# First two w_in blocks of the last layer: gates taken ahead of y's last tile and of waiting weight parts, w_out parts made first, output banks dealt out anew

## The chip, the cores and the metric

The kernel runs on one core of one Trainium2 chip. The metric is the device time of one execution in microseconds (us). Engines are named as in the profile: PE (TensorE, with its weight loads as PEld), DVE (VectorE), ACT (ScalarE), POOL (GpSimd) and SP (SyncE, which issues the transfers).

## The reference

Three stages follow each other. The change lies in the last one.

```
attn = masked softmax attention (2 x 8 heads, 768 positions, 64 wide)     -> x, 1536 x 512
h    = max(x @ w1, x @ w2, x @ w3)                                       1536 x 768
y    = h @ w_out                                                         1536 x 512
h2   = y @ w_in                                                          1536 x 2048
g    = h2 * sigmoid(1.702 * h2)
out  = g @ w_out2                                                        1536 x 512
```

## The kernel before

**Numbers as two parts.** Every matrix that PE multiplies is held as a high part (a rounded copy) and a low part (the number less its high part). One product is three matmuls: high by high, high by low, low by high. For each operand ACT (or POOL) makes the copy, and DVE (or POOL) the difference.

**y.** y is made in 16 tiles, n = 0 to 15 (two batches of 768 rows, four chunks, two halves), each into one of PSUM's banks 0 to 3 in turn. `y_hi(n)` on ACT (L863) copies the tile rounded, `y_raw_copy(n)` on ACT (L868) copies it plain, `y_lo(n)` on DVE (L1151) takes the difference, and after it the bank is free. The sixteenth, n = 15, is y's last tile.

**The last layer.** It goes through 16 blocks n (`MIXES`), eight slices of w_in for each batch. One block is a 2 x 2 block product done by a scheme with seven products in place of eight: `up2(n, 0)` to `up2(n, 6)` on PE (L1393 to L1395, six matmuls each), into two half banks in turn (banks 5 and 6), so that `up2` of product m waits until the product two before it has been read. What reads them:

- `first_copy(n)` on ACT (L900) copies product 0, and `mix(n, 0)` to `mix(n, 6)` on DVE (L1209) add products 1 to 6 up. Four of the mixes give the four tiles of h2.
- `sigmoid(n, w)` on ACT (L907), `gate(n, w)` on DVE (L1214), `g_hi(n, w)` on ACT (L914) and `g_lo(n, w)` on DVE (L1219), w = 0 to 3, make the tiles of g from them. sigmoid(n, 0) needs mix(n, 2), sigmoid(n, 1) mix(n, 4), sigmoid(n, 2) mix(n, 5), sigmoid(n, 3) mix(n, 6).
- `out2(n, u)` on PE (L1492 to L1494, three matmuls each), u = 0 to 11, multiplies g by w_out2 and adds into the six output tiles, which have a bank each in `acc`. The first three need g_lo(n, 0), the next three g_lo(n, 1), and so on. PE puts out2 of block n - 1 between the products of block n: `OUT_SPREAD` says how many behind each product (2, 2, 2, 2, 1, 2, 1). The tiles come in the order 3, 4, 5, 0, 1, 2, 3, 4, 5, 0, 1, 2.

The first block's products are made between y's last four tiles: up2(0, 5) and (0, 6) come right behind y's tile 15. Then come block 1 and its neighbours.

**The weights of a block.** w_in's slice is loaded by SP (L485) and POOL adds up four sums of its quarters (L669, named s1, s3, s2 and s4; s2 needs s1, s4 needs s2). The seven parts have a high and a low part: `in2_hi(n, w)` on ACT (L884; for blocks 0 and 1 POOL does it, L524) and `in2_lo(n, w)` on POOL (L678). Part 1 is s2, part 5 is s4. The two w_out2 slices of a block are loaded by SP (L491) and split by `out2_hi(g)` on ACT (L892) and `out2_lo(g)` on POOL (L683), g = 2n and 2n + 1.

**Orders.** All five engines run lists written out by hand, each in order, with semaphores between them. From block 2 on (and in the kernel before from block 1 on) ACT's list for block n is: sigmoid(n - 1, 3), first_copy(n), g_hi(n - 1, 3), in2_hi(n + 1, 1 to 4), out2_hi(2n) and (2n + 1), in2_hi(n + 1, 5 and 6), for n = 2 to 5 a copy `y_sum_hi` (L873), in2_hi(n + 2, 0), and then sigmoid and g_hi (n, 0 to 2). POOL's is: in2_lo(n + 1, 1 to 4), s4 of block n + 1, out2_lo(2n) and (2n + 1), in2_lo(n + 1, 5 and 6), and then s1, in2_lo(n + 2, 0), s3 and s2 of block n + 2. DVE's is: gate(n - 1, 3), g_lo(n - 1, 3), mix(n, 0), for n = 1 to 4 a sum `y_sum` (L1189), mix(n, 1), for n = 3 to 6 `y_sum_lo` (L1194), mix(n, 2), mix(n, 3), gate(n, 0), mix(n, 4), g_lo(n, 0), gate(n, 1), mix(n, 5), g_lo(n, 1), gate(n, 2), mix(n, 6), g_lo(n, 2).

For block 0 DVE's list behind y's tile 14 is: mix(0, 2 to 4), gate(0, 0), y_lo(15), g_lo(0, 0), gate(0, 1), mix(0, 5), g_lo(0, 1), mix(0, 6), gate(0, 2), g_lo(0, 2).

Of the kernel before, what the change touches and what calls it, by code (L numbers as in the profile page):

```python
# [5 lines left out]
def lsh_attention_ffn(nc, q, k, v, proj, w1, w2, w3, w_out, w_in2, w_out2, out):  # L6
# [5 lines left out]
    B, H, S, D = q.shape  # L12
# [87 lines left out]
    with ctx:  # L100
# [118 lines left out]
        all_banks = [psS[0][:, 0, :], psS[0][:, 1, :], psS[1][:, 0, :], psS[1][:, 1, :],  # L219
                     psR[0][:, :], psR[1][:, :], psR[2][:, :], psO[:, :]]  # L220
        psY = all_banks[0:4]
        acc = all_banks[0:4] + [psR[0][:, :], psO[:, :]]
        psU = [psR[1][:, 0:HALF], psR[2][:, 0:HALF]]

        consts_set = sem("consts_set")
# [287 lines left out]
        def _(pool):  # L513
# [167 lines left out]
            def out2_lo(g):  # L681
                pool.wait_ge(out2_hi_made, g + 1)
                pool.tensor_tensor(w2_parts[:, g % W2_SLOTS, 1, :], out2_raw(g), f32(w2_parts[:, g % W2_SLOTS, 0, :]),  # L683
                                   ALU.subtract).then_inc(out2_split, 1)
# [24 lines left out]
                in2_lo(n, 6)  # L709
            in2_first_sums(2)  # L710
            for n in range(1, MIXES):
                if n + 1 < MIXES:
                    for which in range(1, 5):
                        in2_lo(n + 1, which)
                    in2_last_sum(n + 1)
                out2_lo(2 * n)
                out2_lo(2 * n + 1)
                if n + 1 < MIXES:
                    in2_lo(n + 1, 5)
                    in2_lo(n + 1, 6)  # L720
                if n + 2 < MIXES:
                    in2_first_sums(n + 2)
# [3 lines left out]
        def _(act):  # L726
# [197 lines left out]
            for n in range(2 * OUTS * B):  # L924
                if n == 0:
                    act.wait_ge(h_lo_made, 2 * UPS)
                if n == 2 * OUTS:
                    act.wait_ge(h_lo_made, 2 * UPS * B)
                if n == 2 * OUTS * B - 6:
                    act.activation(table_probe[:, :], ident[:, 0:1], ACT.Sigmoid)  # L930
                if n == 2 * OUTS * B - 1:
                    sigmoid(0, 0)
                y_hi(n)
                y_raw_copy(n)
                if n in (2 * OUTS, 2 * OUTS + 1):
                    for t in T_ORDER2[2 * (n - 2 * OUTS):2 * (n - 2 * OUTS) + 2]:
                        y_sum_hi(0, t)
                if n == 2 * OUTS * B - 4:
                    first_copy(0)
                    out2_hi(0)  # L940
                    out2_hi(1)
            g_hi(0, 0)
            sigmoid(0, 1)
            g_hi(0, 1)
            sigmoid(0, 2)
            g_hi(0, 2)

            for n in range(1, MIXES):
                sigmoid(n - 1, 3)
                first_copy(n)  # L950
                g_hi(n - 1, 3)
                if n == FPS2 + 1:
                    copy_result(0, COPIES[0][2])
                if n == 1:
                    in2_hi(2, 0)
                if n + 1 < MIXES:
                    for which in range(1, 5):
                        in2_hi(n + 1, which)
                out2_hi(2 * n)
                out2_hi(2 * n + 1)  # L960
                if n + 1 < MIXES:
                    in2_hi(n + 1, 5)
                    in2_hi(n + 1, 6)
                if 2 <= n < 6:
                    y_sum_hi(1, T_ORDER2[n - 2])
                if n + 2 < MIXES:
                    in2_hi(n + 2, 0)
                for which in range(3):
                    sigmoid(n, which)
                    g_hi(n, which)  # L970
                if n == FPS2:
                    copy_result(0, COPIES[0][0])
                    copy_result(0, COPIES[0][1])
# [7 lines left out]
        def _(dve):  # L981
# [255 lines left out]
            mix(0, 3)  # L1237
            mix(0, 4)
            gate(0, 0)
            y_lo(2 * OUTS * B - 1)  # L1240
            g_lo(0, 0)
            gate(0, 1)
            mix(0, 5)
            g_lo(0, 1)
            mix(0, 6)
            gate(0, 2)
            g_lo(0, 2)
# [34 lines left out]
        def _(pe):  # L1282
# [195 lines left out]
            def out2(n, u):  # L1478

                b, (i, tile_) = n // FPS2, OUT_UNITS[u]  # L1480
                first, last = n % FPS2 == 0 and u < NT, n % FPS2 == FPS2 - 1 and u >= NT
                if u % TH == 0:
                    pe.wait_ge(g_lo_made, 4 * n + u // TH + 1)
                if u == 0:
                    pe.wait_ge(out2_split, 2 * n + 2)
                if first and b == 0:
                    pe.wait_ge(y_lo_made, 2 * OUTS * B)
                    pe.wait_ge(y_raw_made, 2 * OUTS * B)
                if first and b > 0:
                    pe.wait_ge(*result_done(b - 1, tile_))  # L1490
                wh, wl = w2_parts[:, (2 * n + i) % W2_SLOTS, 0, :], w2_parts[:, (2 * n + i) % W2_SLOTS, 1, :]
                pe.matmul(acc[tile_], g_part(n, i, 0)[:, ts(tile_, P)], wh, start=first, stop=False)  # L1492
                pe.matmul(acc[tile_], g_part(n, i, 0)[:, ts(tile_, P)], wl, start=False, stop=False)  # L1493
                pe.matmul(acc[tile_], g_part(n, i, 1)[:, ts(tile_, P)], wh, start=False, stop=last).then_inc(tile_summed, 1)  # L1494
# [52 lines left out]
```

## Time and profile before

| | us |
|---|---|
| median of 3 runs | 685.02 |
| lowest, highest | 684.53, 685.94 |
| the profiled execution, its own time | 683.02 |
| its span | 681.2 |
| PE busy | 665.6 |
| DVE busy | 493.1 |
| POOL busy | 475.6 |
| ACT busy | 342.7 |

The profile is of one execution. The span runs from its first to its last instruction; some 1.8 us of its own time lie around the span. Matmuls are pipelined: one of 384 columns is shown 0.33 us long, and the next starts about 0.17 us behind it. An engine's idle time stands in brackets behind the instruction that ended it, with the event that released it by the profile. Where several events were waited for, the one named may not be the last.

### The profile page before, as it was taken

The page shows a single profiled execution, that of the slowest core. Times are in us where ns is not written, and L with a number is a line of the kernel's source. Part 1 is how long each engine was busy: PE and PEld are TensorE (multiplying, and loading weights), DVE is VectorE, ACT ScalarE, POOL GpSimd, SP SyncE. Part 2 cuts the span into 40 slices and gives each one's busy share as a digit, 9 for nine tenths or more (in the row PEclk, how much of TensorE's full clock was granted, in tenths as well). Part 3 has the DMA queues.
Part 4 walks back from the last instruction along what each step waited for, and adds up shares of the span by engine and source line. Part 5 has one row for each costly group of instructions (what it writes and reads, how often), then busy time and mean ns, then how long its engine had stood idle before and what let it go on. Part 6 is the DMA issues. An engine that isn't in the chain of part 4 may idle for free.

```text
span 681.2 us, 11928 instructions
## 1 busy us (share of the span) xinstructions
PE 665.6 (98%) x3874; PEld 576.3 (85%) x3874; DVE 493.1 (72%) x971; ACT 342.7 (50%) x752; POOL 475.6 (70%) x542
## 2 busy tenths in 40 slices
PE   7899999999999999999999999989999999999998
PEld 5677777767777789999999999869989889898986
DVE  5778788787877799879788963566777666555554
ACT  3777877777777731011103453455555555545433
POOL 4756757688976899968870538888888767777720
PEclk9999999999999999999999999999999999999999
DMA  5845737548243101111010201122222115222102
GB/s 115 192 94 138 170 89 174 127 121 185 57 124 120 33 23 40 32 32 32 25 46 25 94 0 44 50 62 64 76 78 93 64 50 167 63 63 62 39 25 92
DMA packets 58701, 54.12 MB, mean 79 GB/s; under 512 B 28945, under 2 KB 47633, under 8 KB 58641
## 3 DMA queue, kind: packets, MB, share of 16 engines
q1 hardware_dynamic: 58320, 53.36, 29.1%
q8 instruction: 32, 0.52, 0.3%
q14 instruction: 29, 0.23, 0.1%
q10 hardware_dynamic: 320, 0.01, 0.0%
HBM read 32.51 MB, written 3.15 MB: 52 GB/s over the span
## 4 chain that ended last, share of the span: by engine, by line
PE 92%; DVE 2%; POOL 2%; DMA 1%; issue 1%; ACT 1%; SPq 0%; DVEq 0%; ACTq 0%; POOLq 0%
PE psS L1325 10%; PE psO L1347 9%; PE psR L1333 9%; PE psR L1393 8%; PE psR L1394 8%; PE psR L1395 8%; PE psS L1393 6%; PE psS L1394 6%; PE psS L1395 6%; PE psS L1494 4%; PE psS L1493 4%; PE psS L1492 4%; PE psR L1294 2%; PE psR L1494 1%; PE psR L1493 1%; PE psO L1493 1%
## 5 line engine op out<-in xcount | busy, mean ns | idle before, releaser
L549 POOL TENSOR_SCALAR probs<-probs,lone,inv 128x768 f32<-128x768 f32 x96 | 94.0, 986 | 60.2 <-DVE inv L1010 60.2
L678 POOL TENSOR_TENSOR w_lo<-w_raw,w_hi 128x256 fp32r<-128x256 f32 x96 | 79.7, 842 | 49.7 <-ACT w_hi L884 48.7
L992 DVE TENSOR_REDUCE neg_max<-psS 128x1 f32<-128x768 f32 x96 | 91.2, 951 | 12.3 <-PE psS L1325 9.1
L741 ACT ACTIVATE probs<-psS,neg_max 128x768 f32<-128x768 f32 x96 | 86.5, 901 | 20.7 <-DVE neg_max L992 20.7
L524 POOL TENSOR_SCALAR w_hi<-w_raw 128x256 fp32r<-128x256 f32 (+1 forms) x82 | 50.4, 618 | 51.3 <-PE psS L1395 29.7
L1333 PE MATMUL psR<-ident,probs 128*128 128x128 f32 x576 | 74.7, 273 | 2.3 <-ACT w_raw L734 1.0
L750 ACT ACTIVATE probs_t<-psR 128x384 f32<-128x384 f32 x128 | 59.5, 491 | 31.3 <-PE psR L1333 31.3
L1333 PEld LDWEIGHTS psR<-ident,probs 128*128 128x128 f32 x576 | 66.6, 140 | 6.9 <-POOL probs L549 3.8
L1347 PE MATMUL psO<-probs_t,v_raw 128*64 128x384 f32 x384 | 68.8, 494 | 0.0
L1214 DVE TENSOR_TENSOR v_raw<-v_raw,bits 128x384 f32<-128x384 f32 x64 | 50.0, 782 | 13.9 <-ACT bits L907 11.8
L1393 PE MATMUL psR<-x_hi,w_hi 128*128 128x384 f32 x160 | 53.7, 335 | 4.3 <-POOL w_lo L678 2.7
L1209 DVE TENSOR_TENSOR v_raw<-psR,early 128x384 f32<-128x384 f32 x64 | 35.3, 552 | 30.4 <-PE psR L1395 30.3
L1394 PE MATMUL psR<-x_lo,w_hi 128*128 128x384 f32 x160 | 53.8, 336 | 0.0
L1395 PE MATMUL psR<-x_hi,w_lo 128*128 128x384 f32 x160 | 53.6, 335 | 0.0
L1347 PEld LDWEIGHTS psO<-probs_t,v_raw 128*64 128x64 f32 x384 | 24.9, 136 | 30.9 <-issue 30.6
L884 ACT ACTIVATE w_hi<-w_raw 128x256 fp32r<-128x256 f32 x84 | 30.7, 407 | 35.8 <-POOL w_raw L669 30.1
L907 ACT ACTIVATE bits<-v_raw 128x384 f32<-128x384 f32 x64 | 33.5, 524 | 27.5 <-DVE v_raw L1209 27.3
L683 POOL TENSOR_TENSOR w_parts<-w_raw,w_parts 128x512 fp32r<-128x512 f32 x32 | 40.8, 1296 | 8.4 <-ACT w_parts L892 8.4
L1209 DVE TENSOR_TENSOR early<-psR,early 128x384 f32<-128x384 f32 x48 | 26.5, 553 | 27.6 <-PE psR L1395 27.5
L569 POOL TENSOR_TENSOR w_lo<-w_raw,w_hi 128x256 fp32r<-128x256 f32 x52 | 46.0, 891 | 0.3
L1393 PEld LDWEIGHTS psR<-x_hi,w_hi 128*128 128x128 f32 x160 | 30.0, 188 | 7.6 <-POOL w_lo L678 5.4
L1017 DVE COPY probs_t<-psR 128x384 f32<-128x384 f32 x64 | 35.4, 553 | 0.9 <-PE psR L1333 0.2
(258 smaller groups left out, 1885.0 us busy)
## 6 DMA issues: line engine op xcount, KB each, us to landing
w_raw<-in_moe_w_in SPq DMA_DIRECT2D x16, 512.0 KB, 3.4
w_raw<-in_moe_w_out SPq DMA_DIRECT2D x32, 256.0 KB, 2.6
w_raw<-in_moe_w SPq DMA_DIRECT2D x9, 512.0 KB, 3.8
h_lo<-w_hi SPq DMA_DIRECT2D x22, 192.0 KB, 3.5
h_hi<-w_hi SPq DMA_DIRECT2D x18, 192.0 KB, 3.4
w_raw<-in_q SPq DMA_DIRECT2D x16, 192.0 KB, 3.4
w_raw<-in_k SPq DMA_DIRECT2D x16, 192.0 KB, 4.1
v_raw<-in_v SPq DMA_DIRECT2D x16, 192.0 KB, 2.6
```

The costliest lines, as they stand in the source:

```text
L549: pool.tensor_scalar(probs[i % PROBS][:, :], probs[i % PROBS][:, :], lone[:, i % 6:i % 6 + 1], inv[:, i % 6:i % 6 + 1], ALU.add, ALU.mult) ...
L678: pool.tensor_tensor(in2_slot(w_lo, n, which), in2_raw(n, PARTS2[which]), f32(in2_slot(w_hi, n, which)), ALU.subtract).then_inc(in2_split, 1)
L741: act.activation(probs[i % PROBS][:, :].rearrange("p (a b) -> p a b", a=2), psS[i % 2][:, :, 0:HALF], ACT.Exp, bias=neg_max[:, i % 6:i % 6 ...
L750: act.activation(probs_t[u % 2][:, s // TH, ts(j, TH), ts(s % TH, P)], bank(("probs", i, j))[:, 0:HALF].rearrange("p (c q) -> p c q", c=TH ...
L992: dve.tensor_reduce(neg_max[:, i % 6:i % 6 + 1], psS[i % 2][:, :, 0:HALF], AX.XY, ALU.min).then_inc(max_ready, 1)
L1209: dve.tensor_tensor(o, psU[(7 * n + product) % 2], other, ALU.add).then_inc(mix_added, 1)
L1325: mm = pe.matmul(psS[i % 2][:, j, 0:HALF], stack(n, qs)[0:rows, ts(t, P)], half(stack(n, ks)[0:rows, :], j), start=which == 0, stop=which ...
L1333: mm = pe.transpose(o[:, ts(c, P)], probs[i % PROBS][:, ts(j * TH + c, P)], ident[:, :])
L1347: mm = pe.matmul(psO[a * D:(a + 1) * D, 0:HALF], v_raw[p % 2][a][:, c, :], probs_t[u % 2][:, a, c, :], start=c == 0, stop=c == NT - 1)
L1393: pe.matmul(o, wh, xh, start=c == 0, stop=False)
L1394: pe.matmul(o, wh, xl, start=False, stop=False)
L1395: mm = pe.matmul(o, wl, xh, start=False, stop=c == len(terms) - 1)
```

## The change

It alters only the first two blocks of the last layer, and the banks of the output tiles.

- ACT: sigmoid(0, 1) moves ahead of y_hi(15), and g_hi(0, 0) and g_hi(0, 1) between y_hi(15) and y_raw_copy(15). In block 1, in2_hi(2, 0) and out2_hi(2), out2_hi(3) come first, then sigmoid(1, 0) and g_hi(1, 0), then in2_hi(2, 1 to 4), then sigmoid and g_hi (1, 1) and (1, 2), and last in2_hi(2, 5), (2, 6) and (3, 0).
- DVE: gate(0, 1) moves ahead of g_lo(0, 0), and y_lo(15) moves behind g_lo(0, 1).
- POOL: out2_lo(2) and out2_lo(3) come ahead of in2_lo(2, 1 to 4).
- PE: output tiles 0 to 5 lie in banks 1, 2, 3, 4, 7, 0 (before: 0, 1, 2, 3, 4, 7). The first use of a bank that y has held waits for y's last tile in that bank; a bank that y never held isn't waited for. Before, all of the first six waited for y's last tile.

```diff
--- before.py
+++ after.py
@@ -219,7 +219,9 @@
         all_banks = [psS[0][:, 0, :], psS[0][:, 1, :], psS[1][:, 0, :], psS[1][:, 1, :],
                      psR[0][:, :], psR[1][:, :], psR[2][:, :], psO[:, :]]
         psY = all_banks[0:4]
-        acc = all_banks[0:4] + [psR[0][:, :], psO[:, :]]
+
+        ACC = (1, 2, 3, 4, 7, 0)
+        acc = [all_banks[i] for i in ACC]
         psU = [psR[1][:, 0:HALF], psR[2][:, 0:HALF]]
 
         consts_set = sem("consts_set")
@@ -709,12 +711,16 @@
                 in2_lo(n, 6)
             in2_first_sums(2)
             for n in range(1, MIXES):
+                if n == 1:
+                    out2_lo(2)
+                    out2_lo(3)
                 if n + 1 < MIXES:
                     for which in range(1, 5):
                         in2_lo(n + 1, which)
                     in2_last_sum(n + 1)
-                out2_lo(2 * n)
-                out2_lo(2 * n + 1)
+                if n > 1:
+                    out2_lo(2 * n)
+                    out2_lo(2 * n + 1)
                 if n + 1 < MIXES:
                     in2_lo(n + 1, 5)
                     in2_lo(n + 1, 6)
@@ -930,7 +936,11 @@
                     act.activation(table_probe[:, :], ident[:, 0:1], ACT.Sigmoid)
                 if n == 2 * OUTS * B - 1:
                     sigmoid(0, 0)
+                    sigmoid(0, 1)
                 y_hi(n)
+                if n == 2 * OUTS * B - 1:
+                    g_hi(0, 0)
+                    g_hi(0, 1)
                 y_raw_copy(n)
                 if n in (2 * OUTS, 2 * OUTS + 1):
                     for t in T_ORDER2[2 * (n - 2 * OUTS):2 * (n - 2 * OUTS) + 2]:
@@ -939,20 +949,32 @@
                     first_copy(0)
                     out2_hi(0)
                     out2_hi(1)
-            g_hi(0, 0)
-            sigmoid(0, 1)
-            g_hi(0, 1)
             sigmoid(0, 2)
             g_hi(0, 2)
 
-            for n in range(1, MIXES):
+
+            sigmoid(0, 3)
+            first_copy(1)
+            g_hi(0, 3)
+            in2_hi(2, 0)
+            out2_hi(2)
+            out2_hi(3)
+            sigmoid(1, 0)
+            g_hi(1, 0)
+            for which in range(1, 5):
+                in2_hi(2, which)
+            for which in (1, 2):
+                sigmoid(1, which)
+                g_hi(1, which)
+            in2_hi(2, 5)
+            in2_hi(2, 6)
+            in2_hi(3, 0)
+            for n in range(2, MIXES):
                 sigmoid(n - 1, 3)
                 first_copy(n)
                 g_hi(n - 1, 3)
                 if n == FPS2 + 1:
                     copy_result(0, COPIES[0][2])
-                if n == 1:
-                    in2_hi(2, 0)
                 if n + 1 < MIXES:
                     for which in range(1, 5):
                         in2_hi(n + 1, which)
@@ -961,7 +983,7 @@
                 if n + 1 < MIXES:
                     in2_hi(n + 1, 5)
                     in2_hi(n + 1, 6)
-                if 2 <= n < 6:
+                if n < 6:
                     y_sum_hi(1, T_ORDER2[n - 2])
                 if n + 2 < MIXES:
                     in2_hi(n + 2, 0)
@@ -1237,11 +1259,11 @@
             mix(0, 3)
             mix(0, 4)
             gate(0, 0)
-            y_lo(2 * OUTS * B - 1)
+            gate(0, 1)
             g_lo(0, 0)
-            gate(0, 1)
             mix(0, 5)
             g_lo(0, 1)
+            y_lo(2 * OUTS * B - 1)
             mix(0, 6)
             gate(0, 2)
             g_lo(0, 2)
@@ -1483,9 +1505,9 @@
                     pe.wait_ge(g_lo_made, 4 * n + u // TH + 1)
                 if u == 0:
                     pe.wait_ge(out2_split, 2 * n + 2)
-                if first and b == 0:
-                    pe.wait_ge(y_lo_made, 2 * OUTS * B)
-                    pe.wait_ge(y_raw_made, 2 * OUTS * B)
+                if first and b == 0 and ACC[tile_] < len(psY):
+                    pe.wait_ge(y_lo_made, 2 * OUTS * B - len(psY) + ACC[tile_] + 1)
+                    pe.wait_ge(y_raw_made, 2 * OUTS * B - len(psY) + ACC[tile_] + 1)
                 if first and b > 0:
                     pe.wait_ge(*result_done(b - 1, tile_))
                 wh, wl = w2_parts[:, (2 * n + i) % W2_SLOTS, 0, :], w2_parts[:, (2 * n + i) % W2_SLOTS, 1, :]
```

## Rows read from the trace of the kernel before

**Rows 1.** Page of the profile, head and busy time of each engine
```profile
span 681.2 us, 11928 instructions
...
PE 665.6 (98%) x3874; PEld 576.3 (85%) x3874; DVE 493.1 (72%) x971; ACT 342.7 (50%) x752; POOL 475.6 (70%) x542
```

**Rows 2.** Timeline, engine PE: start us, duration us, engine, line, operation, tiles, [idle before it <-releaser]
```profile
430.67 0.41 PE L1393 MATMUL psR<-x_hi,w_hi 128*128 128x384 f32 x1 [1.63 <-DVE v_raw L1209]
...
438.05 0.33 PE L1393 MATMUL psR<-early_h,w_hi 128*128 128x384 f32 x1
...
446.79 0.41 PE L1393 MATMUL psR<-x_hi,w_hi 128*128 128x384 f32 x1 [1.95 <-POOL w_lo L678]
...
449.50 0.41 PE L1393 MATMUL psR<-x_hi,w_hi 128*128 128x384 f32 x1 [0.73 <-POOL w_lo L678]
...
465.52 0.33 PE L1393 MATMUL psR<-x_hi,w_hi 128*128 128x384 f32 x1
...
481.21 0.33 PE L1393 MATMUL psR<-x_hi,w_hi 128*128 128x384 f32 x1
...
499.44 0.41 PE L1393 MATMUL psR<-early_h,w_hi 128*128 128x384 f32 x1
```

**Rows 3.** Timeline, engine DVE, around y's last tile
```profile
428.98 1.07 DVE L1214 TENSOR_TENSOR v_raw<-v_raw,bits 128x384 f32<-128x384 f32 x1
...
429.98 0.54 DVE L1209 TENSOR_TENSOR v_raw<-psR,early 128x384 f32<-128x384 f32 x1
```

**Rows 4.** Timeline, engine ACT, around y's last tile
```profile
427.38 0.49 ACT L868 ACTIVATE probs_t<-psS 128x384 f32<-128x384 f32 x1
...
427.75 0.53 ACT L914 ACTIVATE h_lo<-v_raw 128x384 fp32r<-128x384 f32 x1
```

**Rows 5.** Timeline, engine DVE, block 1
```profile
439.29 0.56 DVE L1209 TENSOR_TENSOR v_raw<-psR,early 128x384 f32<-128x384 f32 x1 [0.94 <-PE psR L1395]
...
444.85 1.32 DVE L1214 TENSOR_TENSOR v_raw<-v_raw,bits 128x384 f32<-128x384 f32 x1 [4.54 <-ACT bits L907]
...
446.10 0.54 DVE L1209 TENSOR_TENSOR v_raw<-psR,early 128x384 f32<-128x384 f32 x1
...
448.81 0.54 DVE L1209 TENSOR_TENSOR v_raw<-psR,early 128x384 f32<-128x384 f32 x1
...
452.18 0.56 DVE L1219 TENSOR_TENSOR stacks<-v_raw,stacks 128x384 fp32r<-128x384 f32 x1
```

**Rows 6.** Timeline, engine ACT, block 1
```profile
444.31 0.51 ACT L907 ACTIVATE bits<-v_raw 128x384 f32<-128x384 f32 x1
...
453.68 0.40 ACT L884 ACTIVATE w_hi<-w_raw 128x256 fp32r<-128x256 f32 x1
```

**Rows 7.** Timeline, engine POOL, blocks 1 and 2
```profile
439.76 0.74 POOL L678 TENSOR_TENSOR w_lo<-w_raw,w_hi 128x256 fp32r<-128x256 f32 x1 [0.59 <-ACT w_hi L884]
...
442.54 0.74 POOL L669 TENSOR_TENSOR w_raw<-w_raw 128x256 f32<-128x256 f32 x1
...
443.24 1.30 POOL L683 TENSOR_TENSOR w_parts<-w_raw,w_parts 128x512 fp32r<-128x512 f32 x1
...
447.41 1.06 POOL L669 TENSOR_TENSOR sum_of_w<-w_raw 128x256 f32<-128x256 f32 x1
...
454.16 0.81 POOL L678 TENSOR_TENSOR w_lo<-w_raw,w_hi 128x256 fp32r<-128x256 f32 x1 [2.98 <-ACT w_hi L884]
...
457.04 0.74 POOL L678 TENSOR_TENSOR w_lo<-w_raw,w_hi 128x256 fp32r<-128x256 f32 x1
...
457.74 0.74 POOL L669 TENSOR_TENSOR w_raw<-w_raw 128x256 f32<-128x256 f32 x1
```

**Rows 8.** Timeline, engine POOL, the same sum in the two blocks after
```profile
473.72 0.74 POOL L669 TENSOR_TENSOR w_raw<-w_raw 128x256 f32<-128x256 f32 x1
...
489.71 0.74 POOL L669 TENSOR_TENSOR w_raw<-w_raw 128x256 f32<-128x256 f32 x1
```

**Rows 9.** Timeline, engine DVE, last mix of block 4
```profile
498.75 0.54 DVE L1209 TENSOR_TENSOR v_raw<-psR,early 128x384 f32<-128x384 f32 x1
```

## The prediction

> **What bounds the kernel now.** I read the page first. The profiled execution has a span of 681.2 us, and PE is busy for 665.6 of them [rows 1]. So a change of order can win only PE's idle time; no matmul is removed. Then I read PE's timeline from y's last tile to the end, looking for matmuls of 0.41 us in place of 0.33: a longer first one marks a restart after an empty pipe. They stand at the start of three products: up2(1, 0) at 430.67 after 1.63 us idle, up2(1, 6) at 446.79 after 1.95, up2(2, 0) at 449.50 after 0.73 [rows 2]. That is 4.31 us. Behind them PE makes one block in 15.69 us (465.52 to 481.21 are up2(3, 0) and up2(4, 0)), and only one more restart follows, up2(5, 1) at 499.44 [rows 2]. After it there is none up to the end, so whatever PE's start at 499.44 gains, the end gains.
>
> Who ended those idle times? For 430.67 the last event is mix(0, 5) on DVE, 429.98 + 0.54 = 430.52. It was queued behind y_lo(15), g_lo(0, 0) and the 1.07 us of gate(0, 1) [rows 3]. For 446.79 the row names POOL's w_lo, which had long been there; the wait is for mix(1, 4), which ends at 446.64. It stood behind gate(1, 0), which sat 4.54 us waiting for ACT's sigmoid(1, 0) at 444.31 [rows 5, 6]. That sigmoid needs only mix(1, 2) (439.29 + 0.56) [rows 5], but stands behind copies that wait for POOL's s4 sum of block 2, done at 442.54 + 0.74 = 443.28 [rows 7]. For 449.50 it is mix(1, 5), ending at 449.35 [rows 5].
>
> The restart at 499.44 tells more. It follows mix(4, 6), 498.75 + 0.54 = 499.29 [rows 9], and no PE event is in the chain behind that mix. It is a ring of three engines: s4 of block n + 1 (POOL), then copies and sigmoid(n, 0) (ACT), gates and mixes (DVE), g_hi(n, 3) and in2_hi(n + 2, 1) (ACT), four in2_lo and s4 of block n + 2 (POOL). Its beat is read at s4's ends: 458.48 [rows 7], 474.46, 490.45 [rows 8], thus 15.98 and 15.99 us a turn. PE needs 15.69. The ring is slower, PE runs into it, and touches it at 499.44. So 499.44 = 458.48 + 40.96, a path of the ring alone that the change leaves as it is. The question of this change is therefore not how early PE starts, but **how much earlier s4 of block 3 ends than 458.48**.
>
> **The change, part by part.**
>
> *Gates 0 and 1 ahead of y's last tile.* sigmoid(0, 1) moves to before y_hi(15), in time in which ACT waited for y; mix(0, 4), which it needs, is done while that tile still runs, so it costs nothing. g_hi(0, 0) starts where y_raw_copy(15) did, 427.38 in place of 427.75 [rows 4]. So g_lo(0, 0) starts at about 427.93, and because POOL then is in an operation, ends near 428.7; mix(0, 5) follows directly: 428.61 + 0.54 = 429.15, and up2(1, 0) at 429.30 (the 0.15 from mix to matmul as at 430.67). Gain 1.37 of the 1.63 us. y_lo(15) and y_raw_copy(15) are about 1.5 us later; their first reader is now out2(0, 5), which takes bank 3. By the bank order (1, 2, 3, 4, 7, 0) tiles 3 and 4 take banks that y never held, tiles 5, 0, 1, 2 wait for y_lo 13 to 16. In PE's order out2(0, 5) is some 6.5 us behind up2(1, 0), near 435.8, and y_lo(15) ends near 430.7. No wait, no cost; if the banks were dealt as before, out2(0, 0) near 430.3 would wait some 0.4 us. mix(0, 6) must end before up2(1, 1), which is six matmuls of up2 and six of out2 behind 429.30, near 431.8; with g_lo(0, 1) and y_lo(15) ahead of it I get 431.1.
>
> *sigmoid(1, 0) ahead of in2_hi(2, 1 to 6).* up2(1, 3) was at 438.05 [rows 2], its mix(1, 2) 1.24 us later [rows 5]. 1.37 earlier gives 437.92 + 0.56 = 438.48, and sigmoid(1, 0) at 438.52 in place of 444.31. The gate then meets POOL's out2_lo(2), begun near 439.0 and 1.30 us long [rows 7], and ends 0.4 behind it, near 440.7; mix(1, 4) near 441.2. PE wants up2(1, 6) at 446.79 - 1.37 - 1.95 and 0.17 for the lost overlap, 443.3. The 1.95 us go. From mix(1, 4)'s start to mix(1, 5)'s it was 2.71 us [rows 5]; with the four copies that now stand ahead of sigmoid(1, 1) I take 3.3, so mix(1, 5) ends near 444.4: up2(2, 0) can start at 429.30 + 15.69 = 444.99, in place of 449.50. Up to here PE is 4.51 us early.
>
> *POOL, block 1 to the sum s4 of block 3.* POOL does the same instructions, out2_lo(2) and (3) first. I go through its time from y's last tile to 458.48 and change what changes:
> - The 0.59 us before 439.76 [rows 7] (sum, ACT's copy, POOL's difference: a bare latency) is now covered by out2_lo(2): -0.59.
> - The 2.98 us before 454.16 [rows 7] waited for in2_hi(3, 1), 453.68 [rows 6], behind gate and g_hi(1, 3). g_hi(1, 2) now comes one beat of 2.7 us behind mix(1, 5)'s start, near 446.6, g_hi(1, 3) near 449.6: no longer last; s2 of block 3 is. What stays is the same latency, 0.59: -2.39.
> - in2_hi(2, 5) needs s4 of block 2. Formerly the two out2_lo lay between, from 443.24 on [rows 7], and hid that latency. Now POOL goes from s4 straight to in2_lo(2, 5) and waits bare: +0.58.
> - DVE and POOL disturb each other: a POOL sum or difference lasts 0.74 alone (457.04) and 1.06 beside a gate or g_lo (447.41) [rows 7], so +0.32 a meeting. Formerly gate(1, 2), g_lo(1, 2), gate(1, 3), g_lo(1, 3) fell into POOL's 2.98 us of rest. Now POOL does not rest; three meet its work (g_lo(1, 2) falls into the 0.58): +0.96. One meeting less near 429, gate(0, 1): -0.13.
>
> Sum -1.57: s4 of block 3 at 456.9. The Trainium skill, page "SBUF — State Buffer", section "SBUF: two separate sides", says that whichever of a VectorE operation with two SBUF inputs and a GpSimd operation starts first holds the shared port pair for the whole instruction. By that rule each meeting would cost POOL the DVE operation's whole length, not the part that the row shows, and the gain would shrink by some 0.7 us; I take the row.
>
> Bounds. The meetings: free (0) to the whole 0.56 us of an undisturbed g_lo [rows 5], thus a gain of 2.5 down to 0.85. The bare wait: 0, if ACT's copy comes while another DVE operation holds POOL up, to 1.3, if gate(1, 2) loses one more turn (0.70) and in2_hi(2, 5) with it (I have g_hi(1, 2) ready at 446.56 and s4 of block 2 at 446.62, so near that either may be last). Together a gain of 0.15 to 3.1.
>
> *After that.* PE, 4.5 us early, runs into the ring at once: I expect restarts at up2(2, 6) (about 1.4 us), up2(3, 0) (0.9), and small ones at up2(3, 1), up2(4, 1), up2(5, 1). up2(5, 1) starts at 499.44 - 1.57 = 497.87. The stalls that go from block 1 come back in block 2, less 1.57 us. Profiled time 683.02 - 1.57 = 681.45; the runs shown have a median 2.00 above the profiled one, 685.02, so **683.5 us**, -0.23%.
>
> **Rivals.**
> *A: all of PE's 4.5 us stay* (ring not binding). 685.02 - 4.5 = 680.5. For it: the row of releasers shows PE waiting only three times over 0.5 us. Against: it needs s4 of block 3 by 454.0, and POOL, never resting from y's last tile on, would have to lose even its bare latencies and most meetings. 0.12.
> *B: meetings cost the DVE operation's full length.* Three meetings at 0.56 in place of 0.32: gain 0.85, 684.2. Against it stands the row of 1.06 us. It is what the rule quoted above from the Trainium skill, page "SBUF — State Buffer", would make of this case. With the near misses of the bare wait (a gain under 1.2): 0.25.
> *C: slower: in2_hi(2, 5) is late.* It now stands on ACT behind sigmoid and g_hi (1, 1) and (1, 2), whose gates each queue for POOL's turns, two of them 1.3 us long. It is priced one for one: in2_hi(2, 5) later than 446.7 by more than 1.57 makes s4 of block 3 later than before. Four lost turns more (4 x 0.70) give 1.2 us over: 686.3, slower by 0.2%. For it: five gates and differences in a row on that path. Against: POOL idles meanwhile, and then DVE's operations run free at 0.55. 0.09.
>
> **How the numbers follow.** Forecast (gain 1.2 to 2.4) 0.54, A 0.12, B 0.25, C 0.09. The measurement tells 0.2%, 1.37 us, from nothing. Of the forecast's 0.54, about 0.40 lies beyond that; with A, faster 0.52. Slower by over 0.2%: half of C and scatter, 0.08. The same: 0.40. The range leaves out A and the end of C: from 681.6 (gain 3.1 and 0.3 of scatter) to 685.7. The forecast's own: 682.6 to 683.8.
>
> **What would show it.** Right: no idle at up2(1, 6) and up2(2, 0); up2(2, 0) near 445.0; POOL without rest over 0.6 us up to block 3; s4 of block 3 near 456.9; restarts at up2(2, 6) and up2(3, 0); up2(5, 1) about 1.6 us early. Wrong in a step: no restarts in block 2 (A); POOL's operations over 1.2 us beside gates (B); POOL resting over 1 us before in2_lo(2, 5) (C). The forecast falls if the ring's turns in blocks 2 to 4 aren't 15.98 us any more.

## The result, and the profile after

The changed kernel has a median of 682.92 us in 20 runs (681.92 to 684.21), the kernel before 684.00 in 20 runs (682.83 to 685.94). The medians lie 1.08 us apart. The ratio by all runs is 0.998, with a 95% interval of 0.9972 to 0.9988: between 0.8 and 1.9 us faster. Forecast were 683.5 us and -0.23%. The three runs of before that were shown first lay 1.0 us above its median of 20.

The timeline of PE, engine and columns as in [rows 2], which it answers; ahead of it the last matmul of up2(0, 6), and at the end the last matmul of all:

```profile
428.85 0.34 PE L1417 MATMUL psR<-x_hi,w_lo 128*128 128x384 f32 x1
...
429.45 0.41 PE L1415 MATMUL psR<-x_hi,w_hi 128*128 128x384 f32 x1 [0.27 <-DVE v_raw L1231]
...
443.46 0.33 PE L1415 MATMUL psR<-x_hi,w_hi 128*128 128x384 f32 x1
...
445.20 0.33 PE L1415 MATMUL psR<-x_hi,w_hi 128*128 128x384 f32 x1
...
461.04 0.41 PE L1415 MATMUL psR<-x_hi,w_hi 128*128 128x384 f32 x1 [1.74 <-POOL w_lo L680]
...
463.76 0.41 PE L1415 MATMUL psR<-x_hi,w_hi 128*128 128x384 f32 x1 [0.74 <-POOL w_lo L680]
...
466.46 0.41 PE L1415 MATMUL psR<-early_h,w_hi 128*128 128x384 f32 x1
...
498.38 0.41 PE L1415 MATMUL psR<-early_h,w_hi 128*128 128x384 f32 x1
...
676.54 0.39 PE L1516 MATMUL psS<-w_parts,stacks 128*128 128x512 f32 x1
```

up2(1, 0) idles 0.27 us in place of 1.63. up2(1, 6) at 443.46 and up2(2, 0) at 445.20 are 0.33 us long and have no idle time: these two waits are gone, and PE enters block 2 4.3 us earlier than before. Then 1.74 and 0.74 us come back at up2(2, 6) and up2(3, 0), almost what had stood at up2(1, 6) and up2(2, 0), with short restarts at 466.46, 482.42 (not shown) and 498.38. At up2(5, 1) PE is only 1.06 us ahead of 499.44.

The timeline of POOL, answering [rows 7] and [rows 8]:

```profile
439.09 1.30 POOL L685 TENSOR_TENSOR w_parts<-w_raw,w_parts 128x512 fp32r<-128x512 f32 x1
...
445.35 1.06 POOL L671 TENSOR_TENSOR w_raw<-w_raw 128x256 f32<-128x256 f32 x1
...
447.77 0.80 POOL L680 TENSOR_TENSOR w_lo<-w_raw,w_hi 128x256 fp32r<-128x256 f32 x1 [1.36 <-ACT w_hi L890]
...
453.99 0.75 POOL L680 TENSOR_TENSOR w_lo<-w_raw,w_hi 128x256 fp32r<-128x256 f32 x1 [0.59 <-ACT w_hi L890]
...
456.79 0.74 POOL L671 TENSOR_TENSOR w_raw<-w_raw 128x256 f32<-128x256 f32 x1
...
472.70 0.73 POOL L671 TENSOR_TENSOR w_raw<-w_raw 128x256 f32<-128x256 f32 x1
...
488.66 0.73 POOL L671 TENSOR_TENSOR w_raw<-w_raw 128x256 f32<-128x256 f32 x1
```

s4 of block 3 ends at 456.79 + 0.74 = 457.53, in place of 458.48. The rest of 2.98 us is down to the bare 0.59, and a new one of 1.36 stands ahead of in2_lo(2, 5), where 0.58 was expected. s4's next ends are 473.43 and 489.39, turns of 15.90 and 15.96 us.

**One clock for all kernels.** The profiled executions differ by up to 2.7 us before the changed stretch begins. So I count from the start of the last matmul of up2(0, 6), which no edit here moves. For the kernel before it is the first of these two rows of its PE timeline:

```profile
428.70 0.34 PE L1395 MATMUL psR<-x_hi,w_lo 128*128 128x384 f32 x1
...
677.57 0.39 PE L1494 MATMUL psS<-w_parts,stacks 128*128 128x512 f32 x1
```

The last matmul thus starts 248.87 us behind that point before, and 676.54 - 428.85 = 247.69 after: 1.18 us less, in line with the ratio. All profiled executions, counted so (us from that point; "end" is the start of the last matmul). Each row is one execution. Each ratio is against runs of the kernel before on the same chip. Every difference lies inside the interval of its ratio, that of rests_filled_and_y_sums_later at its edge; but the intervals are some 1 to 2 us wide, so a difference of a few tenths between two versions is read from the traces alone:

| kernel | s4 of block 3 ends | up2(5, 1) | end | against before | ratio to before, interval |
|---|---|---|---|---|---|
| before | 29.78 | 70.74 | 248.87 | | |
| changed | 28.68 | 69.53 | 247.69 | -1.18 | 0.998 (0.9972 to 0.9988) |
| y_part_alone | 29.60 | 70.60 | 248.75 | -0.12 | 1.0004 (0.9994 to 1.0015) |
| block1_part_alone | 29.70 | 70.59 | 248.72 | -0.15 | 0.9995 (0.9984 to 1.0005) |
| pool_rests_filled | 27.21 | 68.13 | 246.26 | -2.61 | 0.9962 (0.9949 to 0.9975) |
| three_meetings_more | 29.61 | 70.60 | 248.66 | -0.21 | 0.9998 (0.9988 to 1.0007) |
| y_sums_one_block_later | 28.02 | 68.41 | 246.77 | -2.10 | 0.9957 (0.9944 to 0.997) |
| rests_filled_and_y_sums_later | 26.54 | 66.96 | 245.37 | -3.50 | 0.9936 (0.9922 to 0.9949) |
| banks_as_before | 28.69 | 69.61 | 247.74 | -1.13 | 0.9977 (0.9967 to 0.9986) |
| w_out2_parts_as_before | 28.57 | 69.75 | 247.80 | -1.07 | 0.9986 (0.9976 to 0.9997) |
| gate_ahead_of_g_lo_block1 | 28.21 | 69.14 | 247.27 | -1.60 | 0.9976 (0.9966 to 0.9986) |
| gates_ahead_of_g_lo_all_blocks | 28.71 | 69.66 | 247.88 | -0.99 | 0.9981 (0.9971 to 0.9991) |
| all_three_edits | 26.54 | 66.97 | 245.70 | -3.17 | 0.9958 (0.9944 to 0.9972) |
| mix_right_behind_gate | 26.53 | 65.86 | 243.92 | -4.95 | 0.993 (0.9914 to 0.9945) |

### The profile page after: what moved, and what is told of

The parts are those of the page before. It is cut to its first block, busy times and chain, and to the rows that moved or that the text cites. A ratio compares the mean times of both kernels' runs of the same rounds, so it can differ in the third digit from the quotient of the medians.

```text
span 680.2 us, 11926 instructions
## 1 busy us (share of the span) xinstructions
PE 665.9 (98%) x3874; PEld 576.1 (85%) x3874; DVE 495.7 (73%) x971; ACT 342.8 (50%) x752; POOL 475.2 (70%) x542
## 4 chain that ended last, share of the span: by engine, by line
PE 90%; POOL 3%; DVE 3%; issue 1%; DMA 1%; ACT 1%; SPq 0%; ACTq 0%; DVEq 0%; POOLq 0%
PE psS L1347 10%; PE psO L1369 9%; PE psR L1355 9%; PE psR L1415 8%; PE psR L1416 8%; PE psR L1417 8%; PE psS L1415 6%; PE psS L1417 6%; PE psS L1416 6%; PE psS L1516 4%; PE psS L1515 4%; PE psS L1514 4%; PE psR L1316 2%; POOL w_lo L680 1%; PE psR L1515 1%
```

## The experiments

Theory R is that of the prediction: a ring of POOL, ACT and DVE without PE sets the pace, and the end follows s4 of block 3. Theory S is the plain one: PE's idle times add up, and each one removed is worth itself. A meeting is a POOL operation that runs beside a DVE operation and is longer for it. From "end" less "s4 of block 3" in the table one reads how closely the end follows: for the kernel before, the changed one and the eight single edits other than y_sums_one_block_later it is 219.01 to 219.23 us.

**The change in two halves.** y_part_alone is the kernel before with block 0's part of the change and the new banks; block1_part_alone is the changed kernel with block 0's part taken back:

```diff
                 if n == 2 * OUTS * B - 1:
                     sigmoid(0, 0)
-                    sigmoid(0, 1)
                 y_hi(n)
-                if n == 2 * OUTS * B - 1:
-                    g_hi(0, 0)
-                    g_hi(0, 1)
...
+            g_hi(0, 0)
+            sigmoid(0, 1)
+            g_hi(0, 1)
...
             gate(0, 0)
-            gate(0, 1)
+            y_lo(2 * OUTS * B - 1)
             g_lo(0, 0)
+            gate(0, 1)
             mix(0, 5)
             g_lo(0, 1)
-            y_lo(2 * OUTS * B - 1)
```

> The kernel before with block 0's part of the change only (sigmoid and gate (0, 1) and g_hi (0, 0), (0, 1) ahead, y_lo(15) behind, new banks and waits). Theory R (the ring: the end follows the end of POOL's sum s4 of block 3, which POOL's own list sets): up2(1, 0) starts 1.2 to 1.4 us earlier, the idle time before up2(1, 6) grows from 1.95 to about 3.2 us, s4 of block 3 ends within 0.3 us of its old place and the time falls by 0.1 to 0.3 us. Theory S (PE's idle times add up, each one removed is worth itself): 1.2 to 1.4 us faster.

> The changed kernel with block 0's order on ACT and DVE as before; block 1's orders on ACT and POOL and the new banks stay. Theory R: up2(1, 0) idles its 1.63 us again, sigmoid(1, 0) and all gates of block 1 come 1.2 us later than in the changed kernel, POOL's rest ahead of in2_lo(2, 5) grows from 1.36 to 2 to 2.6 us, and the time lies 0.5 to 1.1 us above the changed kernel's, 0 to 0.6 below the kernel before. Theory S: block 1's two idle times (1.95 and 0.73 us) are gone for good, 2.7 us faster than before.

PE of y_part_alone, at up2(1, 6):

```profile
448.17 0.41 PE L1395 MATMUL psR<-x_hi,w_hi 128*128 128x384 f32 x1 [3.11 <-POOL w_lo L679]
```

The first stall is won as in the changed kernel, and the second grows from 1.95 to 3.11 us. The end gains 0.12 us, where S wants 1.2 to 1.4. POOL of block1_part_alone, at in2_lo(2, 1) and in2_lo(2, 5):

```profile
445.73 0.81 POOL L680 TENSOR_TENSOR w_lo<-w_raw,w_hi 128x256 fp32r<-128x256 f32 x1 [1.36 <-ACT w_hi L890]
...
451.33 0.81 POOL L680 TENSOR_TENSOR w_lo<-w_raw,w_hi 128x256 fp32r<-128x256 f32 x1 [1.36 <-ACT w_hi L890]
```

It rests 1.36 us twice (I had expected one longer rest); the end gains 0.15 us, where S wants 2.7. Each half alone is worth next to nothing, both together 1.18: the first half brings ACT's and DVE's work in block 1 forward, and only then does POOL, with block 1's order, find it done. S falls.

**POOL's rests filled.** The new order on POOL for n = 1, and in2_hi(3, 0) ahead of g_hi(1, 2) on ACT (the semaphore counts of these parts are exchanged to match):

```diff
+                if n == 1:
+                    pool.wait_ge(in2_split, 18)
+                    in2_first_sums(3)
+                    in2_lo(2, 5)
+                    in2_lo(2, 6)
+                    continue
                 if n + 1 < MIXES:
                     in2_lo(n + 1, 5)
...
-            for which in (1, 2):
-                sigmoid(1, which)
-                g_hi(1, which)
+            sigmoid(1, 1)
+            g_hi(1, 1)
+            sigmoid(1, 2)
+            in2_hi(3, 0)
+            g_hi(1, 2)
             in2_hi(2, 5)
             in2_hi(2, 6)
-            in2_hi(3, 0)
```

in2_first_sums(3) is s1, in2_lo(3, 0), s3 and s2 of block 3.

> The changed kernel with POOL's sums s1, s3, s2 and in2_lo(3, 0) of block 3 ahead of in2_lo(2, 5) and (2, 6), and in2_hi(3, 0) on ACT ahead of g_hi(1, 2). POOL's rests of 1.36 us (ahead of in2_lo(2, 5)) and 0.59 (ahead of in2_lo(3, 1)) are filled with work that was due anyway. Theory R: s4 of block 3 ends 1.4 to 1.9 us earlier than in the changed kernel, PE's idle time at up2(2, 6) shrinks by as much, and the time falls by 1.4 to 1.9 us more. Rival (ACT's and DVE's half of the ring, ending in g_hi(1, 3), is what sets the pace): s4 of block 3 moves by less than 0.5 us and the time by as little.

POOL, from s4 of block 2 on; no brackets any more:

```profile
446.72 1.05 POOL L674 TENSOR_TENSOR w_raw<-w_raw 128x256 f32<-128x256 f32 x1
447.74 1.05 POOL L674 TENSOR_TENSOR sum_of_w<-w_raw 128x256 f32<-128x256 f32 x1
...
456.71 0.73 POOL L674 TENSOR_TENSOR w_raw<-w_raw 128x256 f32<-128x256 f32 x1
```

s4 of block 3 ends at 457.44, 27.21 from the common point: 1.47 us earlier than in the changed kernel, and the end 1.43. Moving work that was due anyway into two rests of POOL, an engine that is busy 70% of the time and never named as the bound, gives about as much again as the change itself: 1.43 against 1.18 us by the traces, while the intervals of the two ratios touch. The g_hi rival falls.

**Three more DVE operations in DVE's free time.**

```diff
                 mix(n, 3)
+                if n == 2:
+                    for i in range(3):
+                        if i > 0:
+                            dve.wait_ge(extra_done, i)
+                        dve.tensor_tensor(gap[:, 0:HALF], mix_first, mix_first, ALU.mult).then_inc(extra_done, 1)
                 gate(n, 0)
```

> The changed kernel with three more VectorE operations of 384 columns with two SBUF inputs in block 2, behind mix(2, 3), where DVE is idle for 5 us and POOL makes block 3's parts. They write a tile that nobody reads. Theory R with 0.32 us a meeting: s4 of block 3 ends 0.9 to 1.0 us later and the time rises by as much. Theory R with the whole operation as the price (0.56): 1.7 us. Theory S, or a ring that doesn't bind: DVE has the time, so nothing changes.

The first of the three on DVE, and the operations of POOL that they meet (in2_lo(3, 3), in2_lo(3, 4), s4 of block 3):

```profile
455.55 1.15 DVE L1291 TENSOR_TENSOR gap<-early 128x384 f32<-128x384 f32 x1
```

```profile
456.23 1.06 POOL L681 TENSOR_TENSOR w_lo<-sum_of_w,w_hi 128x256 fp32r<-128x256 f32 x1
457.25 1.05 POOL L681 TENSOR_TENSOR w_lo<-w_raw,w_hi 128x256 fp32r<-128x256 f32 x1
458.26 1.05 POOL L672 TENSOR_TENSOR w_raw<-w_raw 128x256 f32<-128x256 f32 x1
```

Each lasts 1.05 or 1.06 in place of 0.74. s4 ends 0.93 us later and the end is 0.97 later: 0.31 us a meeting. The end by itself is no clean measure in this run. PE idled 2.66 us up to 462.81 for the late s4, and then its granted clock was at half from 464 to 467.5, which put it 1.6 us behind the changed kernel at up2(3, 1). From there it ran without a restart, while the changed kernel waited for its ring at up2(4, 1) and (5, 1), and so the lag shrank to 1.07. What shows the price is s4 itself: in block 3 it ends ahead of that stretch of slow clock, and in block 5 it is 0.96 us late.

By the Trainium skill's page "SBUF — State Buffer", section "SBUF: two separate sides", the pair of ports that DVE and POOL share is held for the whole instruction. That one operation holds up the other, the rows bear out; the price that POOL pays here is 0.31, not the 0.56 that an undisturbed DVE operation is shown with. The DVE operation for its part is shown until 0.4 us behind POOL's end: 1.15 us long here, and 1.58 for gate(1, 0) of the changed kernel beside out2_lo(2), 1.30 long:

```profile
439.22 1.58 DVE L1236 TENSOR_TENSOR v_raw<-v_raw,bits 128x384 f32<-128x384 f32 x1
...
444.69 1.12 DVE L1241 TENSOR_TENSOR stacks<-v_raw,stacks 128x384 fp32r<-128x384 f32 x1
445.73 1.09 DVE L1236 TENSOR_TENSOR v_raw<-v_raw,bits 128x384 f32<-128x384 f32 x1
```

**y's sums one block later.** The sums of y for the second batch and their parts, the long side operations of DVE and ACT in these blocks, move one block back.

```diff
-                if n < 5:
-                    y_sum(1, n - 1)
+                if 2 <= n < 6:
+                    y_sum(1, n - 2)
...
-                if 3 <= n < 7:
-                    y_sum_lo(1, n - 3)
+                if 4 <= n < 8:
+                    y_sum_lo(1, n - 4)
...
-                if n < 6:
-                    y_sum_hi(1, T_ORDER2[n - 2])
+                if 3 <= n < 7:
+                    y_sum_hi(1, T_ORDER2[n - 3])
```

> The changed kernel with the sums of the second batch's y (y_sum, y_sum_hi, y_sum_lo) one block later each. They are DVE operations of 768 columns with two SBUF inputs and cost POOL 0.7 us each in the ring. Up to s4 of block 5 the ring has four of them in place of six. Theory R: s4 of block 3 ends 0.7 us earlier, s4 of block 5 1.4 us earlier, the restart at up2(5, 1) goes, later blocks get the operations back where the ring had half a us to spare, and the time falls by 1.0 to 1.4 us. If PE's start of block 2 sets the end, or the y sums are just DVE work in DVE's free time: no change.

> Both of the last two edits: POOL's rests filled, and y's sums one block later. Theory R: they lie one behind the other on the same path and add up: 1.4 and 1.0 to 1.4, thus 2.4 to 2.8 us below the changed kernel, 3.6 to 4.0 below the kernel before; PE's idle time in block 2 is all but gone. If each only uncovers the same next limit (PE's start of block 2, 4.5 us ahead of before): no more than 3.5 below before.

Alone 0.92 us below the changed kernel, a little less than expected. s4 of block 3 is 0.66 us earlier, s4 of block 5 1.32, and up2(5, 1) 1.12; restarts now stand behind it, at up2(6, 1) (513.05) and at an out2 of 558.84. That the first of them comes from the sums that moved there is not shown. With the filled rests the two add up: 0.92 + 1.43 = 2.35, measured 2.32. That is short of the 2.4 to 2.8 expected, and 3.50 below before is just what the rival allowed, so the time does not tell the two apart. s4 of block 3 does: 1.47 and 0.66 us alone, 2.14 together, and PE keeps one idle time of 0.58 us in block 2.

**Pieces of the change taken back.** Banks dealt as before with the wait for all of y, and out2_lo(2) and (3) behind s4 again:

```diff
-        ACC = (1, 2, 3, 4, 7, 0)
+        ACC = (0, 1, 2, 3, 4, 7)
...
-                if first and b == 0 and ACC[tile_] < len(psY):
-                    pe.wait_ge(y_lo_made, 2 * OUTS * B - len(psY) + ACC[tile_] + 1)
+                if first and b == 0:
+                    pe.wait_ge(y_lo_made, 2 * OUTS * B)
```

> The changed kernel with the output tiles in banks 0, 1, 2, 3, 4, 7 and all first uses waiting for y's last tile again. Theory R: out2(0, 0) waits about 0.5 us for y_lo(15), which is 1.5 us later than it was, PE shows a restart there and is 0.5 us later up to block 2, where the ring swallows it: no change of the end (under 0.2 us). Theory S: 0.5 us slower than the changed kernel.

```diff
-                if n == 1:
-                    out2_lo(2)
-                    out2_lo(3)
...
-                if n > 1:
-                    out2_lo(2 * n)
-                    out2_lo(2 * n + 1)
+                out2_lo(2 * n)
+                out2_lo(2 * n + 1)
```

> The changed kernel with out2_lo(2) and (3) on POOL behind s4 of block 2 again; ACT's new order stays. Theory R: POOL rests 2.5 us ahead of in2_lo(2, 1), for which ACT's copy stands behind sigmoid and g_hi (1, 0), and no longer ahead of in2_lo(2, 5); s4 of block 3 ends 0.8 to 1.4 us later than in the changed kernel, about where it was before the change, and PE idles some 2 us at out2(1, 0) for out2_lo(3), which the ring swallows. Time 0.8 to 1.4 us above the changed kernel. Theory S: the 2 us at out2(1, 0) add to the time on their own, 2 us or more slower.

PE at out2(0, 0) with the old banks:

```profile
432.49 0.47 PE L1514 MATMUL psS<-w_parts,h_lo 128*128 128x512 f32 x1 [0.31 <-DVE h_lo L1173]
```

The wait is there (0.31 us idle, 0.48 with the lost overlap), and PE is 0.57 us later at up2(2, 0). At the end 0.05 are left. With the old place of out2_lo, in the order of time: gate(1, 0) on DVE, in2_lo(2, 1) on POOL, and out2(1, 0) on PE:

```profile
439.90 0.56 DVE L1232 TENSOR_TENSOR v_raw<-v_raw,bits 128x384 f32<-128x384 f32 x1
```

```profile
441.41 0.74 POOL L680 TENSOR_TENSOR w_lo<-w_raw,w_hi 128x256 fp32r<-128x256 f32 x1 [1.60 <-ACT w_hi L886]
```

```profile
446.77 0.34 PE L1413 MATMUL psR<-x_hi,w_lo 128*128 128x384 f32 x1
...
449.15 0.47 PE L1510 MATMUL psR<-w_parts,stacks 128*128 128x512 f32 x1 [2.04 <-POOL w_parts L685]
```

PE idles 2.04 us for out2_lo(3), as expected, loses 1.6 more at half clock (last section), and the ring swallows nearly all of it: the end is 0.11 us later than in the changed kernel, so S is wrong once more. PE has no restart behind that one, so here it reaches the end by its own pace, 0.2 us behind what s4 of block 3, 0.11 earlier, would give. But my own number was wrong too. s4 of block 3 doesn't come 0.8 to 1.4 us later but 0.11 earlier. With POOL at rest, gate(1, 0) lasts 0.56 us in place of 1.58, so ACT's copy comes sooner and the rest ahead of in2_lo(2, 1) is 1.60, not 2.5; and the 1.36 ahead of in2_lo(2, 5) is gone, since out2_lo stands there. The early w_out2 parts are worth nothing in the end's time: they trade one rest for another. Nor are the new banks worth anything. Both hold while the ring is slower than PE; in the last version below, where PE waits for nobody, neither was taken back.

**The order of gates and g_lo.** First in block 1 only, g_lo(1, 1) behind gate(1, 2); then in all blocks, gate(n, w + 1) ahead of g_lo(n, w):

```diff
                 gate(n, 0)
                 mix(n, 4)
-                g_lo(n, 0)
                 gate(n, 1)
+                g_lo(n, 0)
                 mix(n, 5)
-                g_lo(n, 1)
                 gate(n, 2)
+                g_lo(n, 1)
                 mix(n, 6)
                 g_lo(n, 2)
```

> The changed kernel with g_lo(1, 1) behind gate(1, 2) on DVE, in block 1 only. In the changed kernel's trace g_lo(1, 1) comes 0.04 us behind a POOL operation and waits its length, and gate(1, 2) behind it one more, so that g_hi(1, 2) and in2_hi(2, 5) are late and POOL rests 1.36 us in place of 0.58. Theory R: gate(1, 2) ends about 1.0 us earlier, POOL's rest falls to about 0.6, s4 of block 3 and the end come 0.5 to 0.8 us earlier. Rival (POOL loses as much to the meetings that it now does not escape): under 0.3 us.

> The changed kernel with gate(n, w + 1) ahead of g_lo(n, w) on DVE in all blocks from 1 on. Each turn of the ring then passes fewer DVE operations that wait for POOL. Theory R: a turn falls from 15.9 to under 15.0 us in blocks 2 to 4, PE keeps one restart in block 2 (1.0 to 1.4 us at up2(2, 6)) and none behind it; 2.0 to 2.8 us faster than the changed kernel. Rival: POOL's own work with its meetings fills a turn (14.8 us), g_lo comes late for out2, and the gain stays under 1 us.

> POOL's rests filled, y's sums one block later, and gates ahead of g_lo in all blocks. Theory R: PE has no restart over 0.3 us behind up2(1, 0); what is left to win of PE's idle time is won, 4.5 to 5.0 us below the kernel before (3.4 to 3.8 below the changed one). Rival: as with two edits, 3.5 below before.

In block 1 the lost turn was the cause of the long rest. gate(1, 2), and in2_lo(2, 5) behind it:

```profile
445.84 0.65 DVE L1236 TENSOR_TENSOR v_raw<-v_raw,bits 128x384 f32<-128x384 f32 x1 [0.59 <-ACT bits L913]
```

```profile
447.69 0.74 POOL L680 TENSOR_TENSOR w_lo<-w_raw,w_hi 128x256 fp32r<-128x256 f32 x1 [0.59 <-ACT w_hi L890]
```

The gate lasts 0.65 in place of 1.09 and the rest is 0.59 in place of 1.36. s4 of block 3 gains 0.47 us and the end 0.42, a little less than the 0.5 expected; of the rest of the 0.77, 0.26 is paid back in a meeting that POOL now doesn't escape (in2_lo(2, 5) and (2, 6) take 1.76 us together in place of 1.50). In all blocks the edit failed: nothing gained (0.19 us later than the changed kernel), and as a third edit on top 0.33 later than two. Even block 1's gain is gone there: POOL's rest ahead of in2_lo(2, 5) is 1.36 again. Here are DVE's gate(3, 1), g_lo(3, 0), mix(3, 5) and gate(3, 2) with all three edits:

```profile
475.85 0.65 DVE L1246 TENSOR_TENSOR v_raw<-v_raw,bits 128x384 f32<-128x384 f32 x1 [0.59 <-ACT bits L922]
476.42 1.09 DVE L1251 TENSOR_TENSOR stacks<-v_raw,stacks 128x384 fp32r<-128x384 f32 x1
477.44 0.54 DVE L1241 TENSOR_TENSOR v_raw<-psR,early 128x384 f32<-128x384 f32 x1
...
478.57 0.66 DVE L1246 TENSOR_TENSOR v_raw<-v_raw,bits 128x384 f32<-128x384 f32 x1 [0.59 <-ACT bits L922]
```

The gate is short now, but mix(3, 5) stands behind the 1.09 us of g_lo(3, 0), and the next sigmoid needs that mix. From gate to gate it is 2.72 us, as before; the beat of the ring stayed at 15.26 and 15.97 us. So the last run puts each mix right behind its gate, on top of filled rests and later y sums:

```diff
                 gate(n, 0)
                 mix(n, 4)
-                g_lo(n, 0)
                 gate(n, 1)
                 mix(n, 5)
-                g_lo(n, 1)
+                g_lo(n, 0)
                 gate(n, 2)
                 mix(n, 6)
+                g_lo(n, 1)
                 g_lo(n, 2)
```

> POOL's rests filled and y's sums one block later, and on DVE in all blocks from 1 on the order gate 0, mix 4, gate 1, mix 5, g_lo 0, gate 2, mix 6, g_lo 1, g_lo 2: no g_lo between a gate and the mix whose sigmoid is next. The earlier order (g_lo behind the next gate but ahead of the mix) left the ring's turn at 15.26 and 15.99 us, since mix 5 and mix 6 waited for it. Theory R: now a gate follows the one before in 2.0 to 2.3 us in place of 2.7, a turn falls to 14.8 (POOL's own work with its meetings) or less, PE has no restart over 0.3 us behind block 1; 4.2 to 4.9 us below the kernel before. Rival (the ring's turn is POOL's own list, not the steps of ACT and DVE): turns stay at 15.26 and 15.99, 3.5 us below before.

DVE's gate(3, 1), mix(3, 5), g_lo(3, 0), gate(3, 2), then s4 of blocks 3, 4 and 5 on POOL, then PE:

```profile
473.81 0.65 DVE L1246 TENSOR_TENSOR v_raw<-v_raw,bits 128x384 f32<-128x384 f32 x1 [0.59 <-ACT bits L922]
474.38 0.55 DVE L1241 TENSOR_TENSOR v_raw<-psR,early 128x384 f32<-128x384 f32 x1
474.85 0.62 DVE L1251 TENSOR_TENSOR stacks<-v_raw,stacks 128x384 fp32r<-128x384 f32 x1
475.52 0.96 DVE L1246 TENSOR_TENSOR v_raw<-v_raw,bits 128x384 f32<-128x384 f32 x1
```

```profile
454.67 0.74 POOL L674 TENSOR_TENSOR w_raw<-w_raw 128x256 f32<-128x256 f32 x1
...
469.08 0.74 POOL L674 TENSOR_TENSOR w_raw<-w_raw 128x256 f32<-128x256 f32 x1
...
483.52 1.45 POOL L674 TENSOR_TENSOR w_raw<-w_raw 128x256 f32<-128x256 f32 x1
```

```profile
429.49 0.41 PE L1425 MATMUL psR<-x_hi,w_hi 128*128 128x384 f32 x1 [0.26 <-DVE v_raw L1241]
```

From gate to gate 1.71 us, and the turn of the ring from 455.41 to 469.82 is 14.41 us; the next, with s4 of block 5 lengthened to 1.45, is 15.15. Both are shorter than PE's 15.69. The ring's beat was thus not POOL's own list, as the rival had it, but the steps of DVE and ACT. That first matmul of up2(1, 0) is the last restart of PE in the whole trace. 679.6 us against 684.14 of the kernel before on the same chip, ratio 0.993 (0.9914 to 0.9945): this version beats both kernels.

## Why the prediction was right, and where its numbers were off

- *What bounds the kernel* held: only the ring's shift reached the end. Counted from the common point PE entered block 2 4.45 us early (forecast 4.51) and was 1.21 ahead at up2(5, 1) (forecast 1.57). The two halves, the old banks and the old place of out2_lo each moved PE in block 1 by 0.5 us or more, and the end by at most 0.22 other than s4 of block 3. One reading was incomplete: PE has a fifth restart before the change, at up2(2, 1) (452.21, 0.41 us long), so up2(5, 1) was not the only one behind block 1; it is worth 0.2 us and changes nothing in the argument.
- *Block 0*: forecast up2(1, 0) 0.60 us behind up2(0, 6)'s last matmul (429.30 - 428.70); measured 0.60.
- *Block 1*: both waits gone, up2(2, 0) 16.29 behind that matmul by the forecast, 16.35 measured.
- *POOL's sum* was the term that was off: -1.57 forecast, -1.10 measured. The bare wait ahead of in2_lo(2, 5) was 1.36 us, not 0.58, so 0.78 was missing; one meeting fewer (0.3) gave part of it back. The wait was past even the upper bound of 1.3. The step that failed is the comparison of g_hi(1, 2) "ready at 446.56" with s4 of block 2 at 446.62. 446.56 is where g_hi(1, 2) can start. Here is its start in the changed kernel:

```profile
446.86 0.52 ACT L920 ACTIVATE stacks<-v_raw 128x384 fp32r<-128x384 f32 x1 [1.74 <-DVE v_raw L1236]
```

On the clock of the kernel before that is 446.71, 0.15 from the forecast. But the copy in2_hi(2, 5) stands behind it on ACT and starts 0.43 us later still, and POOL 0.48 behind the copy. By the forecast's own times the wait would have been 0.85 us. The rest is the 0.15, and s4 of block 2, which ended 0.36 earlier than forecast. So ACT's copy was held by g_hi, and g_hi by DVE's gate(1, 2). That gate stood behind g_lo(1, 1), which came 0.04 us behind a POOL operation (444.69 against 444.65) and waited its length, and the gate one more; the forecast's beat of 2.7 us had both turns in it. gate_ahead_of_g_lo_block1 shows what they cost: with g_lo(1, 1) out of the way the wait is 0.59.
- *The price of a meeting*, 0.32 from two rows, was 0.31 in three_meetings_more. Rival B falls by it, not by the time: the gain of 1.1 to 1.2 us lies on the border between the forecast's own band (1.2 to 2.4) and the gain under 1.2 that B's chance took in. It came out small by the wait, not by the meetings.
- *The time itself* was met in part by luck. The forecast started from 685.02; from the median of 20 runs, 684.00, the same -1.57 gives 682.43, and 682.92 was measured, 0.49 more. That is the error of POOL's sum.
- *Rival A* (all of PE's 4.5 us) needed the ring not to bind; it was not so here. It is what mix_right_behind_gate comes to, once the ring is made faster: 4.95 us.
- *Rival C* was half true: in2_hi(2, 5) was late, but started 0.4 us behind 446.7 on the clock of before, not the 1.57 that decide the sign.
- *Behind it*: restarts forecast at up2(2, 6), (3, 0), (3, 1), (4, 1), (5, 1); they came there. The ring's turns were 0.11 us shorter in sum than before, so the end gained 1.18 to 1.21 where s4 gained 1.10.

The new order of gates cost 0.33 us more as third edit although up2(5, 1) starts alike (66.97 and 66.96). The traces show where. The products of PE start within 0.02 us of each other up to 557.52, and the next one, at 560.44, is 0.33 later than with two edits. Between them lie the first out2 of the second batch, which wait until DVE and ACT have copied the first batch's output tiles. Those copies stand behind the gates in the lists: DVE's copy of one tile starts at 558.91 in place of 558.52, and PE restarts behind it, here with all three edits:

```profile
558.91 0.69 DVE L1258 COPY results<-psO 128x512 f32<-128x512 f32 x1
...
559.65 0.49 PE L1524 MATMUL psO<-w_parts,h_lo 128*128 128x512 f32 x1
```

No run takes that copy apart from the order of gates. What stays open is how far the last version would gain from the two pieces that are worth nothing here.

## What to carry to other kernels

When the busiest engine waits a few times, look behind the waits for a loop among the other engines that never passes through it, and read its beat. If the beat is slower than the busy engine's own, a wait that is removed ahead of the loop comes back behind it, and only what shifts or shortens the loop counts: here rests of an engine busy 70% of the time, and the order of two DVE operations. In such a loop put the operation that the next engine waits for right behind the one that feeds it, and side work after.

## What was unexpected of the hardware

PE's granted clock can fall to half (from 2.4 to 1.2 GHz) for some 3.5 us behind an idle time in the middle of dense work. In w_out2_parts_as_before, stretches of PE's clock (the third number from the end of a row; columns as named in the first line):

```profile
core 0: us, PE busy (x) PEld busy (x) DVE busy (x) ACT busy (x) POOL busy (x), PEclk, DMA share, GB/s
...
449.00:450.00 1.00, 0.85 (x4) 0.75 (x5) 0.42 (x1) 0.53 (x1) 1.00 (x3) 1.00 0.36 133
450.00:451.00 1.00, 1.00 (x4) 0.81 (x3) 0.99 (x1) 0.00 (x0) 1.00 (x3) 0.51 0.91 193
...
454.00:455.00 1.00, 1.00 (x7) 0.88 (x6) 0.69 (x1) 1.00 (x4) 0.62 (x1) 1.00 0.00 0
```

PE had been idle 2.04 us up to 449.15. The clock is back by 454, having cost PE about 1.6 us (it is 2.2 us behind the changed kernel at 449.15 and 3.9 in block 2), nearly all of which the ring swallowed too. In three_meetings_more it fell likewise, from 464 to 467.5, behind 2.66 us idle. After 1.95 us (before) and 1.74 us (changed) idle it did not fall, nor in y_part_alone after 3.11, so the length of the idle time alone doesn't decide it. The same happens between 12 and 26 us in eight of the fourteen profiled executions, where no edit is. Those eight reach the last matmul of block 0's last product from 429.70 to 431.40 us, the six without it from 428.70 to 429.51. The stretch from 20 to 22 us in all_three_edits, where the kernel before has 1.00 in the clock's column:

```profile
core 0: us, PE busy (x) PEld busy (x) DVE busy (x) ACT busy (x) POOL busy (x), PEclk, DMA share, GB/s
20.00:22.00 2.00, 1.55 (x6) 1.42 (x7) 1.18 (x2) 1.18 (x3) 2.00 (x3) 0.58 0.69 208
```

So a gain of 1 us is better read from a point inside the trace, right ahead of the edit, than from the span.
